# The low parts of the first expert's first weight matrix, made by GpSimd instead of VectorE

## What is computed

```python
logits = x @ w_gate + modality_bias[modality_id]
e_idx = np.argmax(logits, axis=1)
...
for e in range(E):
    mask = e_idx == e
    h = np.maximum(x[mask] @ w1[e], 0.0)
    out[mask] = gate_w[mask, None] * (h @ w2[e])
```

## Time and profile before

| | |
|---|---|
| time, median of 3 runs | 1018.04 us (1016.11 to 1018.49) |
| the profiled execution: time | 1017.2 us |
| the profiled execution: span from first to last instruction | 1015.6 us |
| busy: TensorE, VectorE, ScalarE, GpSimd | 93%, 40%, 31%, 9% |
| the passage: from the last attention matmuls to the first expert matmul | about 230 to 257 us |

### The profile page before, as it was taken

One profiled execution on the slowest core, in us unless ns is written; L12 is line 12 of the kernel. 1 busy time (PEld: TensorE's weight loads), 2 busy tenths in 40 slices (PEclk: granted clock), 3 DMA queues, 4 the chain that ended last, 5 costly groups with the idle time before them and its releaser, 6 DMA issues.

```text
span 1015.6 us, 15686 instructions
## 1 busy us (share of the span) xinstructions
PE 945.2 (93%) x5166; PEld 757.7 (75%) x5166; DVE 408.6 (40%) x1308; ACT 310.2 (31%) x755; POOL 95.3 (9%) x175
## 2 busy tenths in 40 slices
PE   3999999991899999899999939999999999999998
PEld 2777776771788888678888737888888888888887
DVE  4778786866622222442222465312313223123120
ACT  2677676763311111321111333121211211112111
POOL 2111313132000000000000031010100100000000
PEclk9999999995899999999999979999999999999999
DMA  4455646534511111331111031020110200100001
GB/s 102 141 180 171 215 163 225 173 123 157 207 42 45 48 41 41 114 116 49 41 41 41 31 94 51 1 84 1 38 45 0 72 10 0 41 1 11 32 1 42
DMA packets 35987, 76.99 MB, mean 76 GB/s; under 512 B 7520, under 2 KB 9568, under 8 KB 35936
## 3 DMA queue, kind: packets, MB, share of 16 engines
q1 hardware_dynamic: 22048, 49.55, 14.3%
q0 software_dynamic: 6080, 19.93, 6.4%
q10 hardware_dynamic: 7808, 6.87, 2.1%
HBM read 52.74 MB, written 23.59 MB: 75 GB/s over the span
## 4 chain that ended last, share of the span: by engine, by line
PE 92%; DVE 4%; DMA 1%; issue 1%; ACT 1%; POOL 0%; DVEq 0%; ACTq 0%; POOLq 0%
PE bank L627 23%; PE bank L629 22%; PE bank L628 22%; PE bank L482 5%; PE bank L524 5%; PE bank L494 5%; PE bank L501 2%; PE bank L654 2%; PE bank L513 2%; PE bank L698 1%; PE bank L622 1%; DMA limits_i<-in_window 1%; DVE w_lo L1265 0%; DVE masked L991 0%; DVE w_lo L1311 0%
## 5 line engine op out<-in xcount | busy, mean ns | idle before, releaser
L629 PE MATMUL bank<-yT_hi,m_lo 128*128 128x512 f32 x432 | 168.3, 390 | 0.0
L756 ACT ACTIVATE probs<-masked,row_min 128x264 f32<-128x264 f32 (+1 forms) x192 | 93.4, 487 | 77.6 <-DVE row_min L991 77.6
L627 PE MATMUL bank<-yT_hi,m_hi_b 128*128 128x512 f32 x288 | 112.2, 390 | 0.0
L628 PE MATMUL bank<-yT_lo,m_hi_b 128*128 128x512 f32 x288 | 112.2, 390 | 0.0
L1397 DVE TENSOR_TENSOR b_sb<-bank,a_sb 128x512 f32<-128x512 f32 x36 | 24.9, 691 | 187.7 <-PE bank L629 187.7
L629 PEld LDWEIGHTS bank<-yT_hi,m_lo 128*128 128x128 f32 x432 | 81.1, 188 | 16.8
L627 PE MATMUL bank<-w_hi,xT_hi 128*128 128x512 f32 x208 | 84.7, 407 | 9.3 <-DVE w_lo L1265 5.0
L627 PE MATMUL bank<-w_hi,hT_hi 128*128 128x512 f32 x208 | 83.3, 400 | 5.1 <-DVE w_lo L1265 5.1
L915 ACT ACTIVATE gT_hi<-g_sb 128x512 fp32r<-128x512 f32 x36 | 22.8, 632 | 200.1 <-DVE g_sb L1400 200.1
L629 PE MATMUL bank<-w_hi,xT_lo 128*128 128x512 f32 x208 | 83.0, 399 | 0.0
L628 PE MATMUL bank<-w_lo,xT_hi 128*128 128x512 f32 x208 | 82.7, 398 | 0.0
(11 more groups left out here) (189 smaller groups left out, 1562.5 us busy)
## 6 DMA issues: line engine op xcount, KB each, us to landing
w_sb<-in_moe_w SPq DMA_DIRECT2D x4, 2048.0 KB, 9.2
xr<-x_sorted POOLq DMA_DIRECT2D x28, 256.0 KB, 3.0
y_sorted<-y ACTq DMA_DIRECT2D x26, 256.0 KB, 2.0
kT<-in_k_t SPq DMA_DIRECT2D x16, 400.0 KB, 4.1
qT<-in_q_t SPq DMA_DIRECT2D x16, 384.0 KB, 3.4
v_in<-in_v_p SPq DMA_DIRECT2D x16, 384.0 KB, 2.9
out<-o_sb SPq DMA_DIRECT2D x24, 256.0 KB, 2.0
m_sb<-in_moe_w SPq DMA_DIRECT2D x6, 768.0 KB, 6.3
```

Of the source, the lines that this page charges most:

```text
L627: pe.matmul(psum, a_hi, b_hi, start=first, stop=False)
L628: pe.matmul(psum, a_hi, b_lo, start=False, stop=False)
L629: return pe.matmul(psum, a_lo, b_hi, start=False, stop=last)
L756: last = act.activation(probs[n % 2][:, hd, 0:win_of(t)], masked[n % 2][:, hd, 0:win_of(t)], ACT.Exp, bias=row_min[:, n % 2, hd:hd + 1], s ...
```

## The change

The four subtractions that make `w1_lo` of the first expert leave VectorE and go to GpSimd. The first stands behind the last scatter and a wait for `counts_ready`, ahead of the wait for the landed scatters and of the load of `xr0`. The other three stand behind that load and ahead of all that leads to the load of `xr1`; between them and it GpSimd also waits until all four chunks are written and raises `w1_split`.

```diff
@@ block.gpsimd
             for t in range(QT):
                 scatter(B - 1, t)
 
+            def split_first_w1(c):
+                pool.wait_ge(w1_hi_made, c + 1)
+                pool.tensor_tensor(w1_lo[:, c, :], w1_sb[:, c, :], w1_hi[:, c, :].bitcast(F32), ALU.subtract
+                                   ).then_inc(w1_lo_made, 1)
+
+            pool.wait_ge(counts_ready, 1)
+            split_first_w1(0)
             pool.wait_ge(x_scattered, 16 * NT)
             pool.wait_ge(first_pad, 16)
             pool.dma_start(xr[0][:, :], x_sorted[0:P, :]).then_inc(x_loaded[0], 16)
+            for c in range(1, 4):
+                split_first_w1(c)
+            pool.wait_ge(w1_lo_made, 4)
+            pool.sem_inc(w1_split, 1)
             pool.wait_ge(pads_written, 16 * (E - 1))
             pool.wait_ge(tables_ready, 1)
@@ block.vector
-            dve.wait_ge(w1_loaded, 32)
-            for c in range(4):
-                dve.wait_ge(w1_hi_made, c + 1)
-                dve.tensor_tensor(w1_lo[:, c, :], w1_sb[:, c, :], w1_hi[:, c, :].bitcast(F32), ALU.subtract
-                                  ).then_inc(w1_lo_made, 1)
-            dve.wait_ge(w1_lo_made, 4)
-            dve.sem_inc(w1_split, 1)
             keep_xT(0, 0)
```

## The result

The changed kernel takes 1024.66 us (median of 6 runs, 1020.87 to 1025.27), beside 1017.8 us for the kernel before (6 runs, 1016.11 to 1019.26). The ratio is 1.0063, 95% interval 1.0045 to 1.0082: slower by 0.6%, some 6.4 us. The profiled execution has a span of 1023.0 us (time 1024.59), 7.4 us more than the 1015.6 of before.

A forecast was written before the change was run, and what follows sets the result against it. VectorE's w1_lo ahead of xT_lo was taken to hold the first expert matmul. Subtractions blocking VectorE put tables at 257.9 and that matmul at 260.9, 3.6 us later: 1018.0 + 3.6 = 1021.6 us, range 1016.5 to 1025.3.

The forecast's parts named there:

- What bounds the kernel: First expert matmul at 257.27 us waits for VectorE's xT_lo, queued behind w1_lo; removing w1_lo brings at most 2.53 us.
- Behind 257.27 TensorE is busy without a gap: After the first expert matmul, moving its start moves the end by as much, unless something new opens a gap.
- One subtraction, 2.27 us: Cost of one 1024-column subtraction on GpSimd, scaled from a 128x128 multiplication; bounds 1.16 and 3.2 us.
- The gap ahead of the first load hides the first one: First subtraction fits GpSimd's 3.2 us gap between last scatter and xr0's load, costing nothing on GpSimd.
- Standstill: During table building, GpSimd subtractions fully block VectorE operations with two SBUF inputs; 3.6 us later, chance 0.55.
- one cast: A 128x8 VectorE cast overlapping a scatter took 0.37 us, ending within 0.03 us of the scatter's end.
- The sum with the standstill: Tables end at 257.9 instead of 249.97, first matmul at 260.9, 3.6 us later; forecast 1021.6 us.
- Should the arbitration put them in another order, the total stays: While tables are built, the total is four subtractions plus VectorE's remaining work, whatever the interleaving.
- The low-clock stretch moves along unchanged, and the end by as much as the start: TensorE's first 12 matmuls stay at clock 0.50 for 5.14 us; the 3.6 us later start carries to the end.
- The second tile: xr1's load, issued near 258.7, lands in time; as late-tile rival without standstill, +0.4 to +4.2 us, chance 0.22.
- the whole gain: Rival at the first expert matmul: no standstill, no late tile; 1.9 to 2.5 us less, chance 0.15.
- the half-slowed VectorE: Rival during table building: VectorE slowed by half, tables end near 252.5, within 1 us of 1018.0, chance 0.08.

The follow-up runs named there:

- e4: Kernel before, GpSimd unchanged, with VectorE making xT_lo between chunks 1 and 2 of w1_lo; ratio 0.9961 (median 1015.01 us beside 1019.23).
- e1: Changed kernel with only chunk 0 of w1_lo on GpSimd, VectorE making chunks 1 to 3; ratio 1.0012 to the kernel before.
- e6: Kernel before plus 36 appended pairs of GpSimd and VectorE operations; two-input SBUF addition 0.42 us alone, 1.89 beside a subtraction; total time says nothing.
- e3: Changed kernel with chunks 0 and 1 on GpSimd behind the tables, then the second tile's load, then chunks 2 and 3; ratio 1.0027 to the kernel before.
- e5: Kernel before with VectorE making each w1_lo chunk twice, a plain delay without GpSimd work; ratio 1.0041.
- e10: Changed kernel with a small GpSimd fill ahead of the first subtraction and another ahead of the other three; ratio 1.0037 to the kernel before.
- e2: Changed kernel with all four GpSimd subtractions behind the tables, the second tile's load still behind them; ratio 1.0085 to the kernel before.
- e7: Kernel before plus eight appended pairs: rows of three GpSimd subtractions, or a long VectorE operation started first; long addition 1.23 us, subtraction beside it 3.06.

## Why the prediction was right, and where not

The direction, the place and the mechanism in the passage were right, and the time of 1024.66 lies in the range; the forecast of 1021.6 was 3.1 us short. That the range holds it is in part luck: its upper end stood for subtractions of 3.2 us, which took 2.35, and most of what came on top of the forecast, 3.2 of 3.8 us of span, was in none of its terms. By its steps:

- *What bounds the kernel*: right in the passage, shown by e4. But "Behind 257.27 TensorE is busy without a gap" was wrong: the trace of before has four waits of 2.5 us and one of 13.3 behind it, and the four are where the clock fell.
- *One subtraction, 2.27 us*: it took 2.35. *The gap ahead of the first load hides the first one*: on GpSimd, yes; for VectorE e1 shows 2.56 us of harm.
- *Standstill*: right, in the changed kernel, in e1 and alone in e6. The weight I gave it rested on one cast, and the other executions bear that reading out: the same cast ends within 0.04 us of its scatter's end in ten of thirteen, with lengths of 0.33 to 0.40 us, and takes 0.17 in the three (e1, e3, e6) where it begins as the scatter ends.
- *The sum with the standstill*: the term that failed is what VectorE gets done beside the subtractions. I let it work at the boundaries and put the reductions and casts beside the second subtraction, some 1.1 us of work for nothing, and counted 7.9 us for the tables. It was 9.95, because one operation begun inside the load's issue was held through all three subtractions and nothing behind it could run. "Should the arbitration put them in another order, the total stays" was wrong by those 1.1 us; the rest is 0.2 for longer subtractions and some 0.6 by which the two holdings outlasted them. Behind the tables I had counted 3.0 us to the first matmul, and it was 2.52, which made the miss smaller. The first matmul is 5.17 us later, not 3.6.
- *The low-clock stretch moves along unchanged, and the end by as much as the start*: only half right. The first rise gave 0.6 us back, and two more falls later took 3.2. They were in no step of the sum. 4.6 + 3.2 is 7.8, of which 0.4 was given back between the second tile and 575.52 (4.21 left there). The delay without additional falls comes out as 3.2 us of span in e5 and 3.8 in e10, near the forecast of 3.6.
- *The second tile*: issued at 259.36 where I had said 258.7, landed in 3.0 us, never waited for. As a rival it needed the standstill to be absent. e2 has the landing beside the weights, 5.0 us: from 257.5 that would be 262.5, a stand of 2.6 us by estimate, which takes the whole gain of 2.5. What the clock would add to such a stand, no run here shows. My other rivals, the whole gain and the half-slowed VectorE, are ruled out by the rows of the changed kernel and by e6.

## What to carry to other kernels

A gap in GpSimd's row is no free room while VectorE has operations with two SBUF inputs or fast ones from SBUF to SBUF: a subtraction moved there stopped VectorE for its whole length, two times its own VectorE price (2.35 against 1.16 us), and for the whole row where VectorE had begun something inside a DMA issue of GpSimd's. Before moving work to another engine, look whether its consumer needs all of it: putting xT_lo ahead of the two chunks that nobody needs yet brought 0.4% with one moved line. And a delay early on can shrink or grow later where short waits meet the clock: 4.4 us at the first matmul became 3.2 at the end in e5, 5.2 became 7.4 in the changed kernel. Before the end is said to move with the start, look at the granted clock behind every later wait.

## What the runs showed of the hardware that I had not expected

- A VectorE operation that began 0.16 to 0.48 us into the DMA issue of a GpSimd load was held through every subtraction queued behind it: 7.59, 7.55, 7.44, 7.53 and 7.40 us in five cases of three subtractions each, 4.96 with two. One that began 0.15 us in kept its length. In a row without an issue ahead, it went in at the first boundary.
- A running VectorE operation held GpSimd's as well: 3.06 us beside the long addition and 2.78 beside a long multiplication of e7, in place of 2.34.
- The issue of a scatter alone held a cast of 128x8 until its end: 0.37 us in place of 0.17, and 0.33 to 0.40 us in all ten executions, of thirteen, in which it began inside the issue.
- Waits of 2.5 us of TensorE's were followed by full clock in some places and by a fall to 1.2 GHz in others, within one execution and for the same wait in different kernels, at a cost of 1.6 us each.
